# Float32 transposes in both mixtures, with the split into high and low parts moved to the read of PSUM

## The chip, the cores and the metric

The kernel runs on one core of a Trainium2 chip. The metric is the device time of one execution in microseconds; the time of a kernel is the median of its runs.

## The reference, cut to what matters

A causal convolution over 7 taps is followed by two mixtures of experts. x has 4 x 3584 = 14336 rows of 192 numbers; each mixture has 8 experts with w1 of 192 x 1024 and w2 of 1024 x 192. The inputs and the result are float32.

```
# first mixture
do_compute = (x @ w_skip) > 0;  out = x
e = argmax(xc @ w_gate);  gate = softmax(xc @ w_gate)[e]        # xc = x[do_compute]
out[do_compute] = xc + gate * (relu(xc @ w1[e]) @ w2[e])
# second mixture, on the rows that the first one gives
e = argmax(x @ w_gate2 + bias[modality]);  gate = softmax(...)[e]
out = gate * (relu(x @ w1[e]) @ w2[e])
```

## The kernel before, in words

**Stages.** The first stage (lines 353 to 746) convolves, computes the logits and writes every row, with its logits, gate and token number (202 numbers, ROW), to the bucket of its expert in a DRAM tensor. Then `mixture(0)` and `mixture(1)` (lines 751 to 1129) run one after the other. Each goes through the buckets in units of 256 rows. A segment is the run of units of one expert; its first unit (`first`) also converts the weights of the next segment, and in the first mixture computes a product with the next gate (`fold`) between the other matmuls. In this run the first mixture has 33 units in 8 segments, the second 57 units, nearly all in one segment.

**Precision.** The products are taken in fp32r, a form of float32 with fewer bits that TensorE multiplies in one pass. To keep accuracy each operand is split: a high part (the value rounded to fp32r) and a low part (value minus high part), and three of the four products are added up. `xt` holds the transposed rows of a unit in three blocks of 256 columns: block 0 the high part of columns 0 to 127 (DA = 128), block 1 the low part of the same, block 2 the last 64 columns (DB = 64), their high part in partitions 0 to 63 and their low part in partitions 64 to 127.

**One unit g**, engine by engine, each in the order written; semaphores tie them together:

- SyncE (`unit`, line 811): loads the rows of unit g+2 into `ahead` once unit g+1 was split (line 815), then the rows of unit g again into `kept` (line 822, or four columns of them in line 820) once the result buffer is free (`y_read`), and in a first unit, when the weights in `stage` were converted, the weights of the segment after the next (lines 238 to 241, 213, 214).
- ScalarE (`unit`, line 1003): four times `hid_hi`, the relu of an up product read from PSUM (line 1008), in a first unit with pieces of the weights between (line 204). After the fourth, in the first mixture only, `r_copy` (line 995 to 997) copies the finished rows of unit g-1 into `sent`; it waits until the rows sent before have landed in DRAM (`sent_done`). Then `read_xt(g+1)` (line 987) copies the transposed rows from PSUM into `xt`; then `r_exp` (line 1001) for the routing, and `rows_hi(g+2)` (line 991), the high part of the rows in `ahead`.
- VectorE (`unit`, line 1103): four times `hid_lo` (line 1106), in a first unit with low parts of weights (line 208); then in the first mixture `route` (lines 1049 to 1065) and `dest` (lines 1070 to 1075) for the rows of unit g-1, of which line 1060 (`pick`) gives what TensorE needs for the ranks; then `finish(g)` (lines 1084 to 1099), which reads the result from PSUM with the rows in `kept`.
- GpSimd (`unit`, line 872): `split_rows(g+2)`, the low parts (lines 855, 856), then the scatter of the routed rows by indirect DMA (line 862).
- TensorE (`unit`, line 950): 40 matmuls `up` (line 915) once `xt` is ready; `transpose(g+1)` (lines 904, 905, 907); 32 matmuls `down` (lines 924 and 928) in eight steps f of four; in the first mixture `r_ranks(g)` (lines 937, 939) after step 5, in a first unit after step 7. It waits for `rpick_done`, that is for line 1060.

So `transpose(g+1)` stands in the middle of unit g, and what follows it has the time of `down` before `up(g+1)` needs `xt`. `ahead`, `split` and `xt` have one buffer each.

Of the kernel before, what the change touches and what calls it, by code (L numbers as in the profile page):

```python
# [14 lines left out]
def conv_two_moes(nc, x, weight, w_skip, w_gate1, modality, w_gate2, bias2, w1, w2, w2_t, out):  # L39
# [6 lines left out]
    P = 128  # L46
# [29 lines left out]
    with ctx:  # L76
# [73 lines left out]
        ahead = sb("ahead", [P, SUBS, ROW])  # L150
        split = sb("split", [P, SUBS, 2 * D], F32R)
# [599 lines left out]
        def mixture(layer):  # L751
# [5 lines left out]
            with layer_psum:  # L757
# [3 lines left out]
                def s(name):  # L761
                    return sem(f"{name}_{layer}")

                p_h = pb("p_h", [P, HB, 512])
                p_xt = pb("p_xt", [P, 1024], F32R)
# [5 lines left out]
                rows_hi_done, split_done, xt_ready, xt_read = s("rows_hi_done"), s("split_done"), s("xt_ready"), s("xt_read")  # L771
# [30 lines left out]
                with nc.Block() as block:  # L802
                    @block.sync
                    def _(sp):
# [3 lines left out]

                        segs = sp.value_load(n_segs[layer][0:1, 0:1], min_val=2, max_val=E)

                        def unit(g, n, k, slot, first):
                            src = rows_of(g + 2)
                            sp.wait_ge(split_done, g + 2)
                            passed(sp)
                            sp.dma_start(ahead[:, :, :], src).then_inc(ahead_loaded, 16)
# [22 lines left out]
                        sp.dma_start(ahead[:, :, :], rows_of(0)).then_inc(ahead_loaded, 16)  # L838

                        load_weights(sp, sp.value_load(seg_w[layer][0:1, 1:2], min_val=0, max_val=CL - 1))  # L840
                        sp.wait_ge(split_done, 1)
                        sp.dma_start(ahead[:, :, :], rows_of(1)).then_inc(ahead_loaded, 16)
# [7 lines left out]
                    def _(pool):  # L850
                        def split_rows(g):

                            pool.wait_ge(rows_hi_done, g + 1)
                            passed(pool)
                            nc.gpsimd.tensor_tensor(split[:, :, D + DB:2 * D], ahead[:, :, 0:DA], split[:, :, 0:DA].bitcast(F32), ALU.subtract)  # L855
                            nc.gpsimd.tensor_tensor(split[:, :, D:D + DB], ahead[:, :, DA:D], split[:, :, DA:D].bitcast(F32), ALU.subtract)\  # L856
                              .then_inc(split_done, 1)

# [13 lines left out]
                        def unit(g, n, k, slot, first):  # L872
# [7 lines left out]
                            split_rows(g + 2)  # L880
# [8 lines left out]
                        split_rows(0)  # L889
                        split_rows(1)  # L890
# [8 lines left out]
                    def _(pe):  # L899
                        def transpose(g):  # L900
                            pe.wait_ge(split_done, g + 1)
                            for t in range(SUBS):
                                o = t * P
# [78 lines left out]
                    def _(act):  # L982
                        act.preload_act_table(ACT.Exp)

                        def read_xt(g):
                            act.wait_ge(xt_ready, g + 1)
                            nc.scalar.activation(xt[:, :], p_xt[:, 0:3 * UNIT].bitcast(F32), ACT.Copy).then_inc(xt_read, 1)  # L987
# [166 lines left out]
```

## Time and profile before

| | |
|---|---|
| median of 3 runs | 1263.01 us (1259.74 to 1268.81) |
| span of the profiled execution | 1261.0 us |
| mean granted TensorE clock | 0.911 of full speed |
| busy: TensorE / VectorE / ScalarE / GpSimd | 92% / 50% / 39% / 37% |
| up products, line 915 | 461.0 us |
| down products, lines 928 and 924 | 447.2 and 352.4 us |
| transposes, lines 904, 905, 907 | 43.3, 44.7 and 46.1 us |

The profile gives the span of its execution and no device time of its own beside it. Busy times of matmuls that overlap are added up by line, so the lines of TensorE sum to more than its busy time. In the profile PE is TensorE's matmuls, PEld its weight loads, DVE VectorE, ACT ScalarE, POOL GpSimd and SPq the requests that SyncE issues. "idle before <-X" is the time in which the engine had nothing to run before this instruction, and X what ended that.

### The profile page before, as it was taken

What the parts mean: (1) busy time and instruction counts of PE and PEld (TensorE: products, weight loads), DVE (VectorE), ACT (ScalarE), POOL (GpSimd) and SP (SyncE); (2) the same over time, 40 slices, a digit from 0 to 9 for tenths busy, and PEclk for the clock granted to TensorE, in tenths of its full rate; (3) what the DMA queues carried; (4) which work ended last, traced back from release to release, by engine and by line L of the source; (5) the groups of instructions that cost most, each with busy time, mean ns of one, the idle gap of its engine ahead of it and who ended that gap; (6) DMA issues with size and microseconds to landing.
All of it is one profiled execution on the core that took longest, in us unless ns stands there. A gap on an engine that the chain in (4) does not pass through costs nothing. (4 is left out here: it accounts for less than half of the span.)

```text
span 1261.0 us, 27560 instructions
## 1 busy us (share of the span) xinstructions
PE 1154.4 (92%) x8677; PEld 1134.5 (90%) x8678; DVE 625.7 (50%) x1896; ACT 489.1 (39%) x879; POOL 465.4 (37%) x576
## 2 busy tenths in 40 slices
PE   1999998289999999999982999999999999999997
PEld 1998998289999999999982999999999999999997
DVE  1356647426666666666662544444444444444444
ACT  0555545124343444444431433333333333333333
POOL 3177567612332323423331432233332332322334
PEclk7667757559999999999995999999999999999999
DMA  5244434444414334244124311111111111111110
GB/s 122 68 118 136 123 103 117 129 117 106 143 41 135 87 110 119 79 117 118 46 57 132 97 39 45 39 42 42 39 39 45 39 42 42 39 44 40 39 45 27
DMA packets 85561, 97.91 MB, mean 78 GB/s; under 512 B 26719, under 2 KB 76211, under 8 KB 85535
## 3 DMA queue, kind: packets, MB, share of 16 engines
q1 hardware_dynamic: 68362, 67.04, 20.6%
q0 software_dynamic: 15072, 28.47, 6.7%
q10 hardware_dynamic: 2100, 2.09, 0.5%
q8 instruction: 11, 0.18, 0.1%
q14 instruction: 16, 0.12, 0.0%
HBM read 65.79 MB, written 33.54 MB: 79 GB/s over the span
## 5 line engine op out<-in xcount | busy, mean ns | idle before, releaser
L915 PE MATMUL p_h<-xt,w_up 128*128 128x256 f32 x3600 | 461.0, 285 | 13.2 <-ACT xt L987 6.9
L915 PEld LDWEIGHTS p_h<-xt,w_up 128*128 128x128 f32 x3600 | 448.3, 190 | 18.4 <-ACT xt L987 9.2
L928 PE MATMUL p_y<-w_dn,hid_hi 128*128 128x384 f32 (+1 forms) x1440 | 447.2, 371 | 0.2 <-DVE hid_lo L1106 0.2
L1008 ACT ACTIVATE hid_hi<-p_h 128x512 fp32r<-128x512 f32 x360 | 215.0, 598 | 514.5 <-PE p_h L915 512.1
L924 PE MATMUL p_y<-w_dn,hid_lo 128*128 128x192 f32 (+1 forms) x1440 | 352.4, 255 | 0.0
L1106 DVE SCALAR_TENSOR_TENSOR hid_lo<-p_h,hid_hi 128x512 fp32r<-128x512 f32 x360 | 247.1, 690 | 209.2 <-ACT hid_hi L1008 208.7
L924 PEld LDWEIGHTS p_y<-w_dn,hid_lo 128*128 128x128 f32 x1440 | 275.8, 192 | 0.0
L928 PEld LDWEIGHTS p_y<-w_dn,hid_hi 128*128 128x128 f32 x1440 | 272.4, 189 | 1.2 <-DVE hid_lo L1106 0.4
L862 POOL DMA_INDIRECT out<-y_out,idx x114 | 112.3, 985 | 243.9 <-DVE y_out L1099 223.4
L855 POOL TENSOR_TENSOR split<-ahead,split 128x256 fp32r<-128x256 f32 x94 | 64.3, 684 | 300.8 <-ACT split L991 300.7
L455 POOL DMA_INDIRECT buckets<-rows,idx x128 | 125.7, 982 | 68.8 <-issue 50.3
L1092 DVE TENSOR_SCALAR y_lo<-p_y,kept 128x192 f32<-128x192 f32 x114 | 42.3, 412 | 184.2 <-PE p_y L928 184.2
L862 POOL DMA_INDIRECT buckets<-sent,idx x68 | 67.0, 985 | 73.7 <-DVE idx L1075 63.3
L904 PE MATMUL p_xt<-ident_r,split 128*128 128x128 f32 x184 | 43.3, 242 | 40.8 <-POOL split L856 40.8
L987 ACT ACTIVATE xt<-p_xt 128x768 fp32r<-128x768 f32 x92 | 73.9, 803 | 4.7 <-PE p_xt L907 4.7
L208 POOL TENSOR_TENSOR w_dn<-stage,w_dn 128x384 fp32r<-128x384 f32 x44 | 43.3, 1017 | 86.5 <-ACT w_dn L204 86.5
L568 ACT ACTIVATE rows<-p_conv 112x384 f32<-112x384 f32 x64 | 31.0, 493 | 86.4 <-PE p_conv L477 35.5
L904 PEld LDWEIGHTS p_xt<-ident_r,split 128*128 128x128 f32 x184 | 26.1, 142 | 41.3 <-POOL split L856 41.0
L479 PE MATMUL p_conv<-x_in,band 118*112 118x192 f32 x192 | 54.7, 431 | 4.7 <-ACT rows L568 4.7
L991 ACT ACTIVATE split<-ahead 128x384 fp32r<-128x384 f32 x94 | 48.9, 520 | 22.3 <-DMA ahead<-buckets 22.3
L586 ACT ACTIVATE xt<-p_xt 128x1344 fp32r<-128x1344 f32 x32 | 41.3, 1290 | 17.2 <-PE p_xt L492 17.2
L907 PE MATMUL p_xt<-ident_r,split 128*128 128x128 f32 x184 | 46.1, 250 | 0.0
(193 smaller groups left out, 1297.7 us busy)
## 6 DMA issues: line engine op xcount, KB each, us to landing
ahead<-buckets SPq DMA_DIRECT2D x94, 202.0 KB, 2.4
x_in<-in_x SPq DMA_DIRECT2D x16, 672.0 KB
stage<-in_w SPq DMA_DIRECT2D x11, 768.0 KB
kept<-buckets SPq DMA_DIRECT2D x33, 202.0 KB, 2.6
stage<-in_w SPq DMA_DIRECT2D x11, 512.0 KB
stage<-in_w SPq DMA_DIRECT2D x22, 256.0 KB
x_in<-in_w_t SPq DMA_DIRECT2D x9, 512.0 KB, 7.2
x_in<-in_w_t SPq DMA_DIRECT2D x9, 256.0 KB, 8.0
```

The lines of the kernel that those rows point to most:

```text
L455: pool.indirect_dma_start(out=buckets, out_offset=bass.IndirectOffsetOnAxis(ap=idx[:, k, t:t + 1], axis=0), in_=rows[:, k, t, :], in_offse ...
L479: mm = nc.tensor.matmul(o, band[:, head, :], x_in[0:KP, k % 2, :, cols], start=True, stop=True)
L855: nc.gpsimd.tensor_tensor(split[:, :, D + DB:2 * D], ahead[:, :, 0:DA], split[:, :, 0:DA].bitcast(F32), ALU.subtract)
L862: pool.indirect_dma_start(out=to, out_offset=bass.IndirectOffsetOnAxis(ap=place[:, t:t + 1], axis=0), in_=src[:, t, :], in_offset=None, bo ...
L904: nc.tensor.matmul(p_xt[:, o:o + P], split[:, t, 0:DA], ident_r[:, :], start=True, stop=True, is_transpose=True)
L915: mm = nc.tensor.matmul(o, w_up[:, slot, w, f * P:(f + 1) * P], xt[:, a * UNIT:(a + 1) * UNIT], start=(m == 0), stop=(m == len(terms) - 1))
L924: nc.tensor.matmul(p_y[:, t, 0:COLS], hid_lo[:, f, c], w_dn[:, slot, f, 0, 0:COLS], start=False, stop=False)
L928: mm = nc.tensor.matmul(p_y[:, t, 0:2 * COLS], hid_hi[:, f, c], w_dn[:, slot, f, :, 0:COLS], start=(f == 0), stop=(f == FT - 1))
L987: nc.scalar.activation(xt[:, :], p_xt[:, 0:3 * UNIT].bitcast(F32), ACT.Copy).then_inc(xt_read, 1)
L991: nc.scalar.activation(split[:, :, 0:D], ahead[:, :, 0:D], ACT.Copy).then_inc(rows_hi_done, 1)
L1008: nc.scalar.activation(hid_hi[:, 2 * b:2 * b + 2, :], p_h[:, b % HB, :].rearrange("p (f c) -> p f c", f=2), ACT.Relu).then_inc(hi_done, 1)
L1106: nc.vector.scalar_tensor_tensor(hid_lo[:, 2 * b:2 * b + 2, :], p_h[:, b % HB, :].rearrange("p (f c) -> p f c", f=2), 0.0, hid_hi[:, 2 * b ...
```

## The change

The transposes read `ahead` itself, in float32: columns 0 to 127 in one transpose, and a second one of 128 columns that holds the last 64 columns twice. For that `ahead` is loaded with two requests, the second of which writes the last 64 columns again behind the first copy. There are four transposes a unit in place of six. `split`, `rows_hi` and `split_rows` are gone. ScalarE reads the transposed rows into blocks 0 and 2 of `xt`, rounding to fp32r, and VectorE (`xt_lo`, two instructions) then subtracts that from what is in PSUM: into block 1, and in partitions 64 to 127 of block 2. `up(g+1)` now waits for VectorE. `xt_lo(g+1)` stands on VectorE behind the four `hid_lo` and ahead of the gate product's low part, `route`, `dest` and `finish`. SyncE waits for the transposes of unit g+1, and no longer for its split, before it loads `ahead` for unit g+2.

```diff
-        ahead = sb("ahead", [P, SUBS, ROW])
-        split = sb("split", [P, SUBS, 2 * D], F32R)
+        ahead = sb("ahead", [P, SUBS, DA + 2 * DB])
...
-                p_xt = pb("p_xt", [P, 1024], F32R)
+                p_xt = pb("p_xt", [P, 2, UNIT])
...
+                        def load_ahead(src):
+                            sp.dma_start(ahead[:, :, 0:D], src[:, :, 0:D]).then_inc(ahead_loaded, 16)
+                            sp.dma_start(ahead[:, :, D:D + DB], src[:, :, DA:D]).then_inc(ahead_loaded, 16)
...
                         def unit(g, n, k, slot, first):                      # SyncE
                             src = rows_of(g + 2)
-                            sp.wait_ge(split_done, g + 2)
+                            sp.wait_ge(xt_ready, g + 2)
                             passed(sp)
-                            sp.dma_start(ahead[:, :, :], src).then_inc(ahead_loaded, 16)
+                            load_ahead(src)
...
-                        sp.dma_start(ahead[:, :, :], rows_of(0)).then_inc(ahead_loaded, 16)
+                        load_ahead(rows_of(0))
 
                         load_weights(sp, sp.value_load(seg_w[layer][0:1, 1:2], min_val=0, max_val=CL - 1))
-                        sp.wait_ge(split_done, 1)
-                        sp.dma_start(ahead[:, :, :], rows_of(1)).then_inc(ahead_loaded, 16)
+                        sp.wait_ge(xt_ready, 1)
+                        load_ahead(rows_of(1))
...
-                            split_rows(g + 2)                                # GpSimd, and its definition
...
-                        split_rows(0)
-                        split_rows(1)
...
                         def transpose(g):
-                            pe.wait_ge(split_done, g + 1)
+                            pe.wait_ge(ahead_loaded, (g + 1) * 32)
                             for t in range(SUBS):
-                                o = t * P
-                                nc.tensor.matmul(p_xt[:, o:o + P], split[:, t, 0:DA], ident_r[:, :], start=True, stop=True, is_transpose=True)
-                                nc.tensor.matmul(p_xt[:, UNIT + o:UNIT + o + P], split[:, t, D + DB:2 * D], ident_r[:, :], start=True, stop=True,
-                                                 is_transpose=True)
-                                mm = nc.tensor.matmul(p_xt[:, 2 * UNIT + o:2 * UNIT + o + P], split[:, t, DA:DA + 2 * DB], ident_r[:, :],
-                                                      start=True, stop=True, is_transpose=True)
+                                o = slice(t * P, (t + 1) * P)
+                                nc.tensor.matmul(p_xt[:, 0, o], ahead[:, t, 0:DA], ident[:, :], start=True, stop=True, is_transpose=True)
+                                mm = nc.tensor.matmul(p_xt[:, 1, o], ahead[:, t, DA:DA + 2 * DB], ident[:, :], start=True, stop=True, is_transpose=True)
                             mm.then_inc(xt_ready, 1)
...
                         def read_xt(g):                                      # ScalarE
                             act.wait_ge(xt_ready, g + 1)
-                            nc.scalar.activation(xt[:, :], p_xt[:, 0:3 * UNIT].bitcast(F32), ACT.Copy).then_inc(xt_read, 1)
-
-                        def rows_hi(g):
-                            act.wait_ge(ahead_loaded, (g + 1) * 16)
-                            nc.scalar.activation(split[:, :, 0:D], ahead[:, :, 0:D], ACT.Copy).then_inc(rows_hi_done, 1)
+                            whole = xt[:, :].rearrange("p (h c) -> p h c", c=UNIT)
+                            nc.scalar.activation(whole[:, 0:3:2, :], p_xt[:, :, :], ACT.Copy).then_inc(xt_hi_done, 1)
...
-                            rows_hi(g + 2)
-
-                        rows_hi(0)
+
                         read_xt(0)
-                        rows_hi(1)
...
+                        def xt_lo(g):                                        # VectorE
+                            dve.wait_ge(xt_hi_done, g + 1)
+                            nc.vector.tensor_tensor(xt[:, UNIT:2 * UNIT], p_xt[:, 0, :], xt[:, 0:UNIT].bitcast(F32), ALU.subtract)
+                            tail = xt[DB:2 * DB, 2 * UNIT:3 * UNIT]
+                            nc.vector.tensor_tensor(tail, p_xt[DB:2 * DB, 1, :], tail.bitcast(F32), ALU.subtract).then_inc(xt_read, 1)
...
+                            xt_lo(g + 1)
                             if first and not last:
                                 fold_lo(dve, p_fold, 1 - slot, n + 2)
                             if not last:
...
                         nc.vector.memset(valid[:, :], 0.0).then_inc(y_read, 1)
+                        xt_lo(0)
                         segments(dve, unit)
```

## Rows read from the trace of the kernel before

**Rows 1.** Busy time by stretch: length, PE, PEld, DVE, ACT, POOL, PEclk, DMA, GB/s.

```profile
260.10:261.90 1.80, 0.03 (x2) 0.02 (x1) 0.17 (x1) 0.80 (x2) 0.73 (x2) 1.00 0.15 43
262.50:282.90 20.40, 20.40 (x86) 19.78 (x85) 6.54 (x19) 6.58 (x15) 4.96 (x6) 0.50 0.20 57
...
685.00:689.10 4.10, 3.70 (x17) 3.70 (x18) 0.00 (x0) 0.52 (x1) 0.00 (x0) 0.50 0.64 190
...
900.00:1255.00 355.00, 354.03 (x2783) 353.77 (x2781) 153.87 (x327) 128.66 (x222) 111.07 (x145) 1.00 0.14 40
```

**Rows 2.** Transposes: timeline of the weight loads; then by line, ns min/median/max.

```profile
1010.56 0.14 PEld L904 LDWEIGHTS p_xt<-ident_r,split 128*128 128x128 f32 x1
...
1011.09 0.19 PEld L928 LDWEIGHTS p_y<-w_dn,hid_hi 128*128 128x128 f32 x1
...
L904 PEld LDWEIGHTS p_xt<-ident_r,split x184: 137/141/183, 252.2 to 1248.9; 128*128 128x128 f32 x184
L904 PE MATMUL p_xt<-ident_r,split x184: 220/245/368, 252.2 to 1248.9; 128*128 128x128 f32 x184
...
L519 PEld LDWEIGHTS p_log<-ident,mod_f x1: 168/168/168, 7.5 to 7.5; 128*112 128x112 f32 x1
L519 PE MATMUL p_log<-ident,mod_f x1: 461/461/461, 7.5 to 7.5; 128*112 128x128 f32 x1
```

**Rows 3.** Waits from 230 us on: us in total, times, longest.

```profile
ACT sent L997 <- DMA buckets<-sent,idx: 43.0, 15, 7.5
...
PEld p_h L915 <- ACT xt L987: 9.2, 8, 1.8
```

**Rows 4.** Timeline, unit after a first unit: start, duration, engine, line.

```profile
324.41 0.34 SPq L815 DMA_DIRECT2D ahead<-buckets  x1
325.73 0.34 SPq L822 DMA_DIRECT2D kept<-buckets  x1
...
326.71 0.16 DVE L1049 TENSOR_SCALAR valid<-rows 128x2 f32<-128x2 f32 x1
327.88 0.17 DVE L1060 TENSOR_TENSOR pick<-hot,valid 128x16 bf16<-128x16 f32 x1
329.32 0.19 PE L937 MATMUL p_r<-pick,before 128*128 128x24 bf16 x1
330.25 0.54 ACT L997 ACTIVATE sent<-rows 128x404 f32<-128x404 f32 x1 [4.17 <-DMA buckets<-sent,idx]
330.69 0.79 ACT L987 ACTIVATE xt<-p_xt 128x768 fp32r<-128x768 f32 x1
331.54 3.86 PE L915 MATMUL p_h<-xt,w_up 128*128 128x256 f32 x30 [0.70 <-ACT xt L987]
335.61 1.46 PE L915 MATMUL p_h<-xt,w_up 128*128 128x256 f32 x10 [0.22 <-DVE hid_lo L1106]
```

**Rows 5.** The page's costliest groups, with mean ns; last, DMA issues to landing.

```profile
L1008 ACT ACTIVATE hid_hi<-p_h 128x512 fp32r<-128x512 f32 x360 | 215.0, 598 | 514.5 <-PE p_h L915 512.1
L1106 DVE SCALAR_TENSOR_TENSOR hid_lo<-p_h,hid_hi 128x512 fp32r<-128x512 f32 x360 | 247.1, 690 | 209.2 <-ACT hid_hi L1008 208.7
L1092 DVE TENSOR_SCALAR y_lo<-p_y,kept 128x192 f32<-128x192 f32 x114 | 42.3, 412 | 184.2 <-PE p_y L928 184.2
...
kept<-buckets SPq DMA_DIRECT2D x33, 202.0 KB, 2.6
```

**Rows 6.** Timeline of an ordinary unit of the first mixture.

```profile
607.59 0.81 ACT L987 ACTIVATE xt<-p_xt 128x768 fp32r<-128x768 f32 x1
...
609.07 0.17 DVE L1060 TENSOR_TENSOR pick<-hot,valid 128x16 bf16<-128x16 f32 x1
...
610.52 0.19 PE L937 MATMUL p_r<-pick,before 128*128 128x24 bf16 x1
...
611.87 0.76 DVE L1094 SCALAR_TENSOR_TENSOR y_lo<-p_y,kept 128x200 f32<-128x200 f32 x2
```

**Rows 7.** Timeline, start of the second mixture.

```profile
688.52 0.52 ACT L991 ACTIVATE split<-ahead 128x384 fp32r<-128x384 f32 x1 [4.65 <-DMA ahead<-buckets]
```

More of the change, by code:

```diff
@@ L770, in mixture @@
                 ahead_loaded, kept_loaded = s("ahead_loaded"), s("kept_loaded")
-                rows_hi_done, split_done, xt_ready, xt_read = s("rows_hi_done"), s("split_done"), s("xt_ready"), s("xt_read")
+                xt_ready, xt_hi_done, xt_read = s("xt_ready"), s("xt_hi_done"), s("xt_read")
                 h_ready, hi_done, lo_done = s("h_ready"), s("hi_done"), s("lo_done")
@@ L850, in _ @@
                     def _(pool):
[L851 to L857, printed above, removed]
                         def scatter(place, src, to):
```

## The prediction

> **What bounds the kernel now.** I read the busy times by stretch first. In the second mixture TensorE has 354.03 us of work in a stretch of 355 us, at the full clock [rows 1]: only what lies in TensorE's own order moves the time there, and work taken from ScalarE or GpSimd brings nothing. Next the table of waits, for the places where TensorE stands still. In the first mixture ScalarE waits 43.0 us in 15 places for the rows sent to DRAM, and TensorE's weight loads wait 9.2 us in 8 places for ScalarE's copy of the transposed rows [rows 3]. The two belong together, which the timeline shows [rows 4]: in the unit after a first unit the weights of a later expert fill the DMA queues, the sent rows land late, ScalarE stands 4.17 us in `r_copy`, and `read_xt` behind it starts only at 330.69. `up` starts at 331.54, 0.70 us late. This happens after each of the first seven of the eight first units (the eighth loads no weights). The eighth wait is at the start of the second mixture.
>
> **TensorE's part.** Six transposes take from 1010.56 to 1011.09, 0.53 us or 0.088 each [rows 2]. The only float32 transpose in the trace is line 519: one load and one matmul, not two as other float32 products have. Its matmul ends 461 - 168 = 293 ns after its load; at the same low clock the slowest fp32r one (a first one) ends 368 - 183 = 185 ns after [rows 2]. The difference of 108 ns is 128 columns at 1.2 GHz, so float32 takes a second clock per column. At 2.4 GHz that makes 2 x 128 / 2.4 = 107 ns, and four take about 0.45 us: 0.08 us saved a unit. Bounds: if the 0.035 us by which today's transposes exceed 128 columns at 2.4 GHz come on top, four take 0.57 us (0.04 lost); at today's 0.088 they take 0.35 (0.18 saved). I take 0.08, as line 519 is the same instruction. Over the 83 units whose time TensorE sets: **-6.6 us** (-15 to +3).
>
> The Trainium skill (TensorE: Matmul & The Clock Gate, Terms) says that the transpose mode of trn2 is four times faster for FP32. If that means the pace of fp32r, the sum would have the bound of -15 us in this place; line 519's row speaks for half that pace.
>
> **ScalarE and GpSimd.** ScalarE's read has 512 columns in place of 768: 0.60 us by line 1008 for 0.80 [rows 5]. `rows_hi` and `split_rows` go, which TensorE waits for only at the start of a mixture.
>
> **VectorE.** `xt_lo` is two instructions of 256 columns. Between 0.41 us for 192 and 0.69 for 512 columns [rows 5] each takes 0.47; with some overlap 0.9 for both. In an ordinary unit the read starts at 607.59 [rows 6] and now ends at 608.2, `xt_lo` at 609.1. `up` needs `xt` only when `finish` reads the result, at 611.87 [rows 6]: hidden by `down`, in both mixtures; without that cover it would be 0.7 a unit (0.9 more for 0.2 less). But in the first mixture `xt_lo` stands ahead of `route`, whose `pick` TensorE awaits in the middle of `down`: `route` takes 1.17 + 0.17 us to the end of `pick` (326.71 to 328.05) [rows 4], so `pick` is ready at 610.4. TensorE comes for it at 610.52 today and at 610.44 then [rows 6]. It just fits: cost 0, bounds 0 and 0.3 us in each of 18 ordinary units, +5 us at most.
>
> **The unit after a first unit** is where the change costs. There `pick` is ready at 328.05 today, before TensorE comes for it at 329.32, and only `up` has to wait for the late read [rows 4]. Now `route` stands behind `xt_lo`, that behind `read_xt`, that behind `r_copy`. The read ends at 331.3, `xt_lo` at 332.2, `pick` at 333.5. TensorE stands from 329.2 to 333.5 with two steps of `down` still to do. Today `up` could have started 1.5 us after the rank matmuls (331.54 - 0.70 - 329.32). So it starts at 335.0 in place of 331.54: 3.4 us later, in seven units: **+24 us**. The unit that follows loses today about 0.5 us because VectorE is behind with `finish` (30 matmuls take 4.07 us to 335.61, at 0.12 each they need 3.6 [rows 4]); with `up` later this goes: **-3.5 us**.
>
> This rests on the order of the queue. The Trainium skill (TensorE: Matmul & The Clock Gate, Part 1, Architectural detail) says that TensorE pulls only weight loads ahead and keeps its matmuls in program order, and that ScalarE and VectorE are strict FIFO. By that rule nothing of `down` slips past the rank matmuls and the 24 us stand; if it could, only the 0.7 us by which `xt` comes later would be left, 5 us in seven units. The trace agrees as far as it goes: no matmul of `down` is seen ahead of ranks that stand before it.
>
> **The clock.** The new stalls last 4.3 us or more. At 260.10:261.90 TensorE is idle for 1.8 us at clock 1.00, and 262.50:282.90 then runs at 0.50 although it is busy throughout [rows 1]. The stalls of today's seven units, 0.7 to 1.8 us, leave the clock high. So I expect a fall after nearly every new stall. In 685.00:689.10, dense `up` at 0.50, 17 matmuls take 3.70 us [rows 1] where 2.1 would do at 0.12 each: 1.6 us lost before the clock is back at 689. I take 2.0 each, six times: **+12 us** (0 to 7 x 3 = 21).
>
> **SyncE.** The load of `ahead` leaves half a unit earlier than needed, as before; a second request costs the queue about 0.6 us. `kept` now waits behind both. It follows `ahead` by 1.3 us when nothing holds it (324.41 to 325.73) [rows 4] and lands in 2.6 [rows 5]. The transposes end about half a microsecond before the read at 607.59, so `kept` lands at 607.1 + 0.2 + 0.6 + 1.3 + 2.6 = 611.8, and `finish` reads it at 611.87 [rows 6]. In the second mixture `finish` may begin 0.5 us later. Its cover is the next `up`, 5 us; without it, 0.5 a unit. Weights are requested after the same waits as before: 0.
>
> **Start of the second mixture.** ScalarE stands in `rows_hi(1)` until `ahead` lands at 688.52 [rows 7] before it may read the first `hid_hi`; this wait goes, and the first transposes need no split (1.5 us less in the chain, against 0.6 for the second request and 0.7 for `xt_lo`). **-2 us** (0 to -4). In the first mixture the start waits for the gate product's operand anyway: 0.
>
> **Sum** against the span of 1261.0: -6.6 + 24 - 3.5 + 12 - 2 = +24, 1285. The median of the runs lies 2 us above that span; with the same distance the median after is **1287 us**.
>
> **Rivals.** (A) *The wait for the ranks comes, the clock stays high.* For: today's stalls of up to 1.8 us in these units did not lower it. Against: the fall after 1.8 us at 261.9. Sum without 12: **1275**. (B) *Faster.* The sent rows land early: the loads of `ahead` and `kept` at 324.41 and 325.73 are no longer requested beside them. If they land 4.17 us earlier, ScalarE's read is done before TensorE asks for ranks; the new wait is gone, and today's 9.2 us too: -6.6 - 9 - 3.5 - 2 = -21, **1242**. It decides once the rows land over 4 us sooner. Against: in SyncE's order those two stand behind the requests for the weights, so they can hardly have held anything up. (C) *The float32 transposes go in two passes of two clocks*, as other float32 products do: eight of 0.107 a unit, 0.86 in place of 0.53 us, 83 times 0.33 = +27 in place of -6.6: **1321**. Line 519 is a single instruction, which speaks against it. (D) *The ordinary units of the first mixture wait too*, 0.3 us each in 18, and the clock falls in all seven, 3 us each: +5 and +9 more: **1301**.
>
> **Chances.** Forecast 0.55; A 0.2; B 0.08; C 0.03; D 0.14. Two runs of one kernel differ by up to about 1%, which is what a measurement can tell from no change: 12.6 us. Slower by more holds the forecast, C, D and a quarter of A: 0.77. Same: most of A, 0.16. Faster: B, 0.07. The range runs from A with a somewhat larger saving on transposes, 1269, to D, 1303; it leaves out B and C.
>
> **What would show it.** In the profile after: PE L937's line has "idle before" of about 30 us in seven places, each over 4 us, released by DVE `pick`; the wait of PE L915 for `xt` is nearly gone; the clock row shows dips in the first mixture; the second mixture has units of 9.84 us and no idle. The prediction is wrong if those seven stalls are absent, if the transposes' four loads take over 0.57 us, or if the clock stays at 1.00.

## The result, and the profile after

The kernel after takes **1298.51 us** (median of 4 runs, 1294.43 to 1304.26), the kernel before 1263.01: the ratio is 1.0289 (95% interval 1.0244 to 1.0334). A later comparison gave 1.0277 (1.0217 to 1.0337). The forecast of 1287 us had the sign and most of the way there, and the range (1269 to 1303) holds the time; 11.5 us are missing from the point. The profiled execution took 1300.72 us, its span is 1299.0.

The busy time by stretch comes first, as before. The columns are those of [rows 1]; the first fence is of the kernel after, the second, a stretch that the rows ahead of the prediction don't have, of the kernel before.

```profile
282.95:661.83 378.88, 337.85 (x2443) 328.82 (x2441) 230.11 (x794) 125.85 (x255) 80.05 (x82) 0.94 0.33 94
900.00:1255.00 355.00, 355.00 (x2743) 355.00 (x2742) 183.28 (x397) 104.04 (x181) 70.82 (x74) 1.00 0.18 47
293.75:300.58 6.83, 6.29 (x30) 6.28 (x31) 3.96 (x17) 0.60 (x1) 1.96 (x2) 0.50 0.09 30
338.13:341.54 3.41, 3.41 (x17) 3.39 (x16) 2.28 (x10) 0.00 (x0) 1.53 (x2) 0.50 0.08 27
```

```profile
282.95:661.83 378.88, 366.39 (x2822) 356.79 (x2819) 240.14 (x853) 160.47 (x319) 126.83 (x158) 1.00 0.34 97
```

The second mixture is full as before. The first is not: in the same stretch TensorE works 338 us where it had 366, and its clock is 0.94 on average for 1.00. Both short stretches are at half clock: they begin at the end of a stall (the first 0.5 us before it, the second 0.6 us after it), and TensorE is busy in all the rest. There are seven such, 44.4 us in all.

What TensorE waits for is in the table of waits from 230 us on (line waited, us in total, times, longest), with other waits that changed:

```profile
DVE idx L1044 <- DMA kept<-buckets: 168.4, 57, 5.6
...
DVE xt L1065 <- ACT xt L954: 65.6, 36, 6.6
...
ACT sent L960 <- DMA buckets<-sent,idx: 41.5, 8, 6.9
PE p_r L903 <- DVE pick L1020: 38.5, 8, 6.3
...
PE p_h L881 <- issue: 6.0, 7, 1.2
```

The wait of the weight loads of `up` for `read_xt` (9.2 us in 8 places, [rows 3]) is gone in the first mixture; at the start of the second `up` now waits 2.4 us for VectorE's part of `xt`. The ranks' wait for the pick has come: 38.5 us in 8 places, of which 3.48 at the end of the mixture stood there before (3.22). Seven others make 35.0 us, 3.99 to 6.31 each (forecast: about 30, each over 4). The last row, seven waits of `up` for "issue", is one that the prediction does not have.

The second unit of this kind shows the chain. This is the timeline of the kernel after; it answers to [rows 4].

```profile
333.26 0.26 PE L890 MATMUL p_y<-w_dn,hid_lo 128*128 128x200 f32 x1
334.15 0.54 ACT L960 ACTIVATE sent<-rows 128x404 f32<-128x404 f32 x1 [3.94 <-DMA buckets<-sent,idx]
334.60 0.58 ACT L954 ACTIVATE xt<-p_xt 128x512 fp32r<-128x512 f32 x1
335.21 0.42 DVE L1065 TENSOR_TENSOR xt<-p_xt,xt 128x256 fp32r<-128x256 f32 x1 [4.28 <-ACT xt L954]
335.65 0.43 DVE L1067 TENSOR_TENSOR xt<-p_xt,xt 64x256 fp32r<-64x256 f32 x1
336.11 0.17 DVE L1009 TENSOR_SCALAR valid<-rows 128x2 f32<-128x2 f32 x1
...
337.28 0.17 DVE L1020 TENSOR_TENSOR pick<-hot,valid 128x16 bf16<-128x16 f32 x1
...
337.51 0.19 PE L903 MATMUL p_r<-pick,before 128*128 128x24 bf16 x1 [3.99 <-DVE pick L1020]
```

Read it downward: the sent rows land, ScalarE copies, then reads `xt`; VectorE writes the low half; then `route`; then TensorE, idle since 333.52, may go on. Every link is as forecast. The ordinary unit and the transposes, also of the kernel after, answer to [rows 6] and [rows 2]:

```profile
356.55 0.59 ACT L954 ACTIVATE xt<-p_xt 128x512 fp32r<-128x512 f32 x1
...
359.25 0.18 DVE L1020 TENSOR_TENSOR pick<-hot,valid 128x16 bf16<-128x16 f32 x1
...
359.48 0.10 PEld L903 LDWEIGHTS p_r<-pick,before 128*128 128x128 bf16 x1 [0.18 <-DVE pick L1020]
```

```profile
1048.71 0.14 PEld L873 LDWEIGHTS p_xt<-ident,ahead 128*128 128x128 f32 x1
1048.81 0.14 PEld L874 LDWEIGHTS p_xt<-ident,ahead 128*128 128x128 f32 x1
1048.92 0.14 PEld L873 LDWEIGHTS p_xt<-ident,ahead 128*128 128x128 f32 x1
1049.03 0.14 PEld L874 LDWEIGHTS p_xt<-ident,ahead 128*128 128x128 f32 x1
1049.14 0.19 PEld L894 LDWEIGHTS p_y<-w_dn,hid_hi 128*128 128x128 f32 x1
```

The pick comes just as TensorE's matmuls do, and the four transposes take 1049.14 - 1048.71 = 0.43 us, 0.108 each.

**Where the 38.0 us went** (1299.0 - 1261.0), by the distance from the first `up` matmul of a unit to that of the next:

```
                                             before    after  difference
start, to unit 1                             282.87   280.81    -2.1
7 units after a first unit                    80.05   114.45   +34.4
7 first units (of units 3 to 29)             106.41   105.84    -0.6
the other 17 units of 1 to 31                178.16   189.47   +11.3
unit 32, and the change of mixture            37.92    36.81    -1.1
unit 33                                       12.55    11.39    -1.2
units 34 to 88 (9.92, then 9.85 each)        546.00   541.57    -4.4
last unit to the end                          17.04    18.68    +1.6
```

### The profile page after: what moved, and what is told of

It is laid out like the page before. It is cut to its first block and busy times, and to the rows that moved or that the text cites. A ratio compares the mean times of both kernels' runs of the same rounds, so it can differ in the third digit from the quotient of the medians.

```text
span 1299.0 us, 27192 instructions
## 1 busy us (share of the span) xinstructions
PE 1160.5 (89%) x8493; PEld 1140.0 (88%) x8494; DVE 697.7 (54%) x2080; ACT 431.1 (33%) x785; POOL 363.1 (28%) x388
## 2 busy tenths in 40 slices
DMA packets 123161, 103.12 MB, mean 79 GB/s; under 512 B 52286, under 2 KB 113810, under 8 KB 123134
## 5 line engine op out<-in xcount | busy, mean ns | idle before, releaser
L881 PE MATMUL p_h<-xt,w_up 128*128 128x256 f32 x3600 | 467.6, 289 | 10.2 <-issue 6.0
L881 PEld LDWEIGHTS p_h<-xt,w_up 128*128 128x128 f32 x3600 | 458.1, 197 | 13.4 <-issue 7.8
L894 PE MATMUL p_y<-w_dn,hid_hi 128*128 128x384 f32 (+1 forms) x1440 | 455.6, 376 | 0.0
L1044 DVE TENSOR_SCALAR idx<-kept 128x2 int32<-128x2 f32 x57 | 10.3, 180 | 168.4 <-DMA kept<-buckets 168.4
L873 PE MATMUL p_xt<-ident,ahead 128*128 128x128 f32 x184 | 46.7, 280 | 37.0 <-DMA ahead<-buckets 37.0
L1065 DVE TENSOR_TENSOR xt<-p_xt,xt 128x256 fp32r<-128x256 f32 x92 | 38.5, 418 | 65.6 <-ACT xt L954 65.6
L454 PE MATMUL p_conv<-x_in,band 118*112 118x192 f32 x192 | 60.4, 465 | 4.6 <-ACT rows L543 4.6
L873 PEld LDWEIGHTS p_xt<-ident,ahead 128*128 128x128 f32 x184 | 26.2, 142 | 37.4 <-DMA ahead<-buckets 37.2
L954 ACT ACTIVATE xt<-p_xt 128x512 fp32r<-128x512 f32 x92 | 54.3, 591 | 9.0 <-PE p_xt L874 9.0
L454 PEld LDWEIGHTS p_conv<-x_in,band 118*112 118x112 f32 x192 | 44.2, 254 | 7.3 <-ACT rows L543 6.6
L561 ACT ACTIVATE xt<-p_xt 128x1344 fp32r<-128x1344 f32 x32 | 41.3, 1290 | 18.7 <-PE p_xt L467 18.7
L874 PE MATMUL p_xt<-ident,ahead 128*128 128x128 f32 x184 | 46.1, 277 | 0.0
```

Source lines behind the costliest of these rows:

```text
L454: mm = nc.tensor.matmul(o, band[:, head, :], x_in[0:KP, k % 2, :, cols], start=True, stop=True)
L873: nc.tensor.matmul(p_xt[:, 0, o], ahead[:, t, 0:DA], ident[:, :], start=True, stop=True, is_transpose=True)
L874: mm = nc.tensor.matmul(p_xt[:, 1, o], ahead[:, t, DA:DA + 2 * DB], ident[:, :], start=True, stop=True, is_transpose=True)
L881: mm = nc.tensor.matmul(o, w_up[:, slot, w, f * P:(f + 1) * P], xt[:, a * UNIT:(a + 1) * UNIT], start=(m == 0), stop=(m == len(terms) - 1))
L894: mm = nc.tensor.matmul(p_y[:, t, 0:2 * COLS], hid_hi[:, f, c], w_dn[:, slot, f, :, 0:COLS], start=(f == 0), stop=(f == FT - 1))
L954: nc.scalar.activation(whole[:, 0:3:2, :], p_xt[:, :, :], ACT.Copy).then_inc(xt_hi_done, 1)
```

## The experiments

Each ratio is to the kernel before, run beside it on the same chip. In the first group of four (before_wait, pick_first, read_first, before_read_first) the kernel before itself took 1300.63 us, not 1263. The first stage took longer there: in the four traces unit 0 starts at 290 to 295 us, elsewhere at 250 to 257. Why is not shown. Expectations of this group that name absolute times are therefore read as ratios or differences. In the second group it took 1262.52, in the third 1264.30.

The same ledger for all traces, in us:

```
                     7 after first   other 17   units 1-32   one unit of   last unit
                                                             mixture 2     to the end
before                    80.05       178.16      402.5         9.92         17.0
after                    114.45       189.47      446.6         9.85         18.7
before_wait              108.27       182.48      434.9         9.94         17.0
before_read_first         72.75       185.70      401.9         9.92         17.0
read_first                72.42       185.55      400.0         9.85         18.7
pick_first                83.70       175.07      400.6         9.85         18.6
kept_first               112.83       187.06      442.1         9.85         16.2
ranks_late                98.41       195.29      438.9         9.82         18.7
pick_and_read             71.73       178.71      392.1         9.85         17.8
all_three                 71.89       178.50      392.5         9.85         16.2
before_both               71.97       184.64      400.5         9.92         17.1
after_again              110.76       189.79      443.2         9.85         18.7
transposes_twice         110.93       188.14      441.7        10.29         18.7
all_again                 71.46       178.34      391.7         9.85         16.2
```

The rows after and after_again are two executions of the same kernel. They differ by 3.7 us in the first column (and by 6.1 us in the time up to unit 1, which is not in this table), so a difference of that size between two traces says nothing by itself.

**The wait alone, in the kernel before.** Nothing but the new order of waits is added: VectorE may not route before `xt` of the next unit has been read.

```diff
                             if not last:
+                                if not first:
+                                    dve.wait_ge(xt_read, g + 2)
                                 route(g)
```

> The kernel before the change with one wait added: in the units of the first mixture that are no first units, VectorE waits for the read of the transposed rows of the next unit ahead of route. No transposes, loads or splits are changed. Theory: this alone makes most of the loss. pick follows the late read by 1.4 us, seven stalls of about 3.6 us, a fall of the clock after each, 27 us in the units themselves and 5 us in those after them, 1285 to 1298. The rivals (SyncE's requests, float32 transposes) expect no loss beyond what a bare wait costs: 1261 to 1268.

It took 1331.46 us beside 1300.63: ratio 1.0236 (1.0202 to 1.0271). One line of waiting, with the old transposes, reproduces 2.36 of the 2.89%. Here are the wait of the second such unit and the clock in the stretch that begins 0.6 us before the end of this wait:

```profile
372.63 0.20 PE L937 MATMUL p_r<-pick,before 128*128 128x24 bf16 x1 [3.88 <-DVE pick L1060]
```

```profile
372.04:378.87 6.83, 6.24 (x29) 6.23 (x30) 4.46 (x17) 0.97 (x2) 3.04 (x4) 0.50 0.30 88
```

The seven stalls last 2.88 to 4.73 us. A fall comes with six of them; with the shortest, 2.88 us, it does not. This kernel has none of the new transposes, so they are not needed for the clock to fall.

**The pick ahead of `xt_lo`** (VectorE, first mixture, units that are not first):

```diff
-                        def route(g):
+                        def route(g, between=None):
...
                             nc.vector.tensor_tensor(q3(pick1), q3(hot), spread(valid[:, :]), ALU.mult).then_inc(rpick_done, 1)
+                            if between:
+                                between()
...
-                            xt_lo(g + 1)
+                            if first or last:
+                                xt_lo(g + 1)
...
-                                route(g)
+                                route(g, None if first else lambda: xt_lo(g + 1))
```

> In the units of the first mixture that are no first units, xt_lo(g+1) moves behind pick on VectorE; all else as in the changed kernel. Theory (the order on VectorE: ranks wait for pick, pick for xt_lo, xt_lo for the late read, and the clock falls in that stall): pick is ready 2.8 us after the transposes begin, the seven waits of TensorE before the rank matmuls are gone, the clock stays at 1.00 through the first mixture, and the small waits before the first units (0.6 to 1.2 us, line 881, issue) go too. up then waits for the late xt, about 0.75 us more than before the change in seven units. Span 1257 to 1262, median 1259 to 1264. Rival 1 (SyncE's later requests and the two loads of ahead): nothing of them is changed here, so 1290 or more. Rival 2 (float32 transposes pull the clock down): four of them a unit are still there, the falls stay, 1280 or more.

**ScalarE reads `xt` ahead of `r_copy`** (same units):

```diff
-                                if not last and b == NB - 1:
+                                if first and not last and b == NB - 1:
                                     r_copy(g)
...
                             read_xt(g + 1)
+                            if not first and not last:
+                                r_copy(g)
```

> In the units of the first mixture that are no first units, ScalarE reads the transposed rows ahead of r_copy; VectorE keeps the order of the changed kernel. Theory: xt_lo no longer hangs on the rows sent to DRAM, pick is ready about 3.5 us after the transposes begin in every such unit, so the seven stalls and the falls of the clock go, and with them the 0.9 to 1.7 us that up waited for xt already before the change. Span 1244 to 1250, median about 1248: faster than both kernels. If the stalls come from SyncE's requests or from the transposes themselves, they stay: 1280 or more.

Ratios: pick_first 0.9972 (0.9956 to 0.9989), read_first 0.9939 (0.9918 to 0.9960). Either cut of the chain turns the loss of 2.9% into a small gain, and no wait ahead of the ranks is left in either until the mixture's end. pick_first gained 4.8 us, where up to 4 were expected, though the clock still fell once, for 3.4 us. read_first gained 8 us, where 13 to 19 were expected. (Nine of its ten executions took 1289.99 to 1297.83 us; one took 5782.41, and nothing here shows why.) What remains differs. In pick_first `up` still has to wait for `xt`, as in the kernel before and longer: six waits of 1.6 to 2.1 us at this place.

```profile
368.70 6.55 PE L881 MATMUL p_h<-xt,w_up 128*128 128x256 f32 x40 [1.78 <-DVE xt L1069]
```

In read_first that goes too (72.4 us for the seven units), but the pick stays behind `xt_lo`, and the waits for "issue" ahead of first units remain (4.5 us, waits of the trace of read_first, 325 to 690 us):

```profile
PE p_h L881 <- DVE hid_lo L1074: 5.2, 5, 2.1
PE p_h L881 <- issue: 4.5, 7, 0.9
```

**The same order of ScalarE in the kernel before:** the edit of read_first.

> The kernel before the change with r_copy behind the read of the transposed rows on ScalarE in the units of the first mixture that are no first units. It tells how much of a gain of the same edit in the changed kernel is the edit's own. Theory: the waits of up for xt in seven units (8 us together) and what follows them (4 us) go: 1249 to 1253, some 4 us above the changed kernel with the same edit. If the late read is not what up waits for, 1261 to 1264.

Ratio 0.9956 (0.9927 to 0.9985). The seven units after a first one go from 80.05 to 72.75 us; the units behind them give back 7.5 us, because VectorE's `finish` is late instead and `up` waits in its middle for `hid_lo`. By the medians the order gains 6.5 us, half of the 10 to 14 expected; by this ledger hardly any of that lies in the first mixture (402.5 and 401.9 us). The traced execution took 1300.55 us, 6.5 above its median, so its trace may not show the gain; where it lies is open. So ScalarE's order cost the kernel before little; the late copy came to matter when the ranks were tied to it.

**SyncE asks for `kept` first:**

```diff
                         def unit(g, n, k, slot, first):
-                            src = rows_of(g + 2)
-                            sp.wait_ge(xt_ready, g + 2)
-                            passed(sp)
-                            load_ahead(src)
                             src = rows_of(g)
                             sp.wait_ge(y_read, g + 1)
...
+                            src = rows_of(g + 2)
+                            sp.wait_ge(xt_ready, g + 2)
+                            passed(sp)
+                            load_ahead(src)
...
                         segments(sp, unit)
+                        sp.wait_ge(ahead_loaded, (total(sp) + 2) * 32)
+                        passed(sp)
```

> The changed kernel, with SyncE asking for the unit's kept rows ahead of the rows of two units on, in place of behind them. Theory (ranks wait for the pick, pick for xt_lo, xt_lo for read_xt, read_xt for the sent rows): the seven waits ahead of the ranks stay, 4 to 6 us each; only the tail of the second mixture, where the finish waits 2.4 us for kept rows, gets about 1.5 us shorter, so the time is 1 to 2 us under the changed kernel (ratio to it 0.997 to 1.001). Rival (SyncE's queue: kept rows held up by the wait for the transposed rows pace the units): most of the 57 waits of VectorE for kept rows, 5.6 us each, end in shorter units, and the time falls by 15 us or more.

The changed kernel was measured beside it:

> The changed kernel itself, once more, as the one that the others of this group are compared with. Its first comparison gave 1.0289 of the kernel before. The runs so far show the kernel before at 1300.63 us here and at 1263.01 us in the first session, the difference lying in the first stage; if the first stage is all that differs, the loss stays about 36 us and the ratio is 1.028 (1.022 to 1.033).

after_again 1300.30 us, 1.0277 (1.0217 to 1.0337); kept_first 1297.17, 1.0272 (1.0214 to 1.0330). The two cannot be told apart, and the seven stalls are still there (3.6 to 5.3 us), so SyncE's order is not the cause. It is a good case of a large wait that costs nothing. In the kernel after, VectorE waits 168.4 us in 57 places for `kept`. In kept_first (740 to 1290 us) that wait is replaced by one for the matmuls:

```profile
DVE y_lo L1054 <- PE p_y L896: 130.6, 53, 2.5
...
DVE idx L1046 <- DMA kept<-buckets: 5.8, 1, 5.8
```

and the unit stays at 9.85 us. Only the last unit, with no next `up` to cover it, is shorter: 16.25 for 18.68 us.

**Float32 transposes issued twice** (second mixture only):

```diff
-                            for t in range(SUBS):
+                            for t in list(range(SUBS)) * (2 if last else 1):
```

> The changed kernel, with each of the four float32 transposes of a unit issued twice in the second mixture, and once in the first, as before; the output is the same. It measures what these transposes cost on TensorE where nothing else ends the unit. By the spacing of four transposes and the next weight load in the trace (0.43 us a unit), 57 units of the second mixture get 0.43 us longer each: 24.5 us over the changed kernel (units of 10.28 us for 9.85), ratio to it about 1.019. If float32 transposes cost no more than the two-byte ones of before (0.088 us a step), it is 20 us; if each took 0.14 us, 32 us. If the clock fell because of them, the granted clock in the second mixture, 1.00 now, would fall and the loss would be over 40 us.

1326.00 us beside after_again's 1300.30, ratio of the medians 1.0198. Units 34 to 88 take 565.77 in place of 541.57 us: 0.440 a unit, 0.110 a transpose. (The old transposes, which the expectation calls two-byte ones, are fp32r.) The load of each of the eight follows the last by 0.10 to 0.11, and the clock stays up:

```profile
1049.47 0.14 PEld L873 LDWEIGHTS p_xt<-ident,ahead 128*128 128x128 f32 x1
...
1050.23 0.14 PEld L874 LDWEIGHTS p_xt<-ident,ahead 128*128 128x128 f32 x1
1050.34 0.19 PEld L894 LDWEIGHTS p_y<-w_dn,hid_hi 128*128 128x128 f32 x1
```

```profile
740.00:1300.00 560.00, 560.00 (x4357) 560.00 (x4356) 281.74 (x599) 163.28 (x273) 107.49 (x110) 1.00 0.19 48
```

**The ranks always at the end of `down`:**

```diff
-                                if not last and f == (FT - 1 if folds else 5):
+                                if not last and f == FT - 1:
```

> The changed kernel, with TensorE's rank matmuls always behind the last down matmuls of the unit, not behind the sixth of ten. The pick comes at T+8.5 us as before, but four steps of down (2.4 us with the slow clock) are done while TensorE waits. Theory: the seven units after a first one lose 2.1 to 2.4 us each (16 us in all), the wait ahead of the ranks goes from 5.0 to about 3.2 us, and the 0.6 to 1.2 us ahead of the seven first units mostly go, since nothing holds TensorE's sequencer in the middle of down: 15 to 22 us under the changed kernel, ratio to the kernel before 1.010 to 1.016. Rival (the pick is not what TensorE waits for): no wait gets shorter.

1292.73 us, ratio 1.0222 (1.0184 to 1.0261), where the changed kernel had 1.0289 and 1.0277: a gain of some 8 us, half of what was expected. The seven units behave as forecast, 114.45 to 98.41 us (2.3 each), with stalls of 2.3 to 4.05 us ahead of the ranks (3.4 on average), and the clock still falls after each. Against after_again (110.76) the seven gain 1.8 each. The rest of the expectation was wrong. Behind the sixth step stand two more steps of `down`, not four. The waits ahead of first units do not go: they are 0.7 to 1.8 us now, the other 17 units take 5.8 us more, and one first unit 1.5 us more. To move the rank matmuls does not shorten these waits. They go with the pick, which comes 3.99 to 4.53 us after the first transpose, where the changed kernel has 4.0: `up` follows its end by 2.1 or 2.6 us in each of the seven places, against 2.2 or 2.7.

**All three orders together,** and without SyncE's:

> The changed kernel with three orders changed: ScalarE reads xt ahead of the copy that waits for the sent rows (units other than a first one, first mixture), VectorE picks ahead of xt_lo in the same units, and SyncE asks for kept rows first. The first two alone gave 0.9939 and 0.9972 of the kernel before. Theory: each of the two takes away the same link, so together they give hardly more than the better one, and the tail 1 us besides: 0.990 to 0.995 of the kernel before, no wait ahead of the ranks, no fall of the clock after them. Rival (the two links cost separately and add): 0.985 or less.

> all_three without SyncE's order. Against all_three it shows what SyncE's order is worth: by the two tails (16.24 and 18.7 us) 2.4 us, and nothing in the units. Ratio to the kernel before 0.986 to 0.988; the first mixture takes 392 to 394 us from unit 1 to unit 33, the seven units after a first one 10.2 us each, and those ahead of a first one 10.1 to 10.4 us (11.0 to 11.5 in the changed kernel).

> all_three once more, on the chip and beside the runs of the others of this group, for a second comparison with the kernel before. The first gave 0.9852 (0.9797 to 0.9908). Ledger by stages: first mixture 10 us shorter than in the kernel before, second 4.4, tail 0.8, start 0 to 2: 15 to 17 us in all, ratio 0.986 to 0.988.

all_three 1245.69 us, 0.9852 (0.9797 to 0.9908), and again 1250.97, 0.9888 (0.9855 to 0.9921); pick_and_read 1250.80, 0.9884 (0.9838 to 0.9930). It beats both kernels: 1.1 to 1.5% under the kernel before, about 4% under the change as it was made. I had expected hardly more than read_first alone (0.9939), which was wrong; the rival, that the two add up, had 0.985 or less. The two cuts do more together, since each removes what the other leaves: the seven units take 71.9 us, as in read_first, and the other 17 take 178.5, not 185.6. In all_three ScalarE still waits 4.12 us for the sent rows, but nothing of TensorE's stands behind it:

```profile
328.04 0.59 ACT L956 ACTIVATE xt<-p_xt 128x512 fp32r<-128x512 f32 x1
332.74 0.54 ACT L962 ACTIVATE sent<-rows 128x404 f32<-128x404 f32 x1 [4.12 <-DMA buckets<-sent,idx]
```

```profile
333.42 0.17 DVE L1028 TENSOR_REDUCE den<-expd 128x2 f32<-128x16 f32 x1 [2.51 <-ACT expd L966]
```

```profile
337.12 1.46 PE L883 MATMUL p_h<-xt,w_up 128*128 128x256 f32 x10 [0.76 <-DVE hid_lo L1078]
```

```profile
288.00:652.00 364.00, 359.18 (x2745) 352.06 (x2744) 252.97 (x897) 140.76 (x287) 89.99 (x92) 1.00 0.38 104
```

That is the chain as it now stands (ScalarE, VectorE, TensorE, and TensorE's stretch): the late sent rows hold `r_exp` behind `r_copy`, VectorE's `den` waits 2.51 us for it, `finish` and so `hid_lo` are late, and TensorE loses 0.76 us in place of 3.99. The clock stays at 1.00. SyncE's order makes no difference that can be measured: 0.9884 without, 0.9888 with it (in the traces the last unit takes 17.8 and 16.2 us).

**What the change is worth in the right order:** the kernel before with the edits of before_read_first and kept_first. It has the six old transposes and the splits ahead of them, so it prices both together.

> The kernel before (two-byte-step transposes, rows split ahead of them) with two of the three orders of all_three: ScalarE reads xt ahead of the copy that waits for the sent rows, SyncE asks for kept rows first. It shows what the float32 transposes are worth once the orders are right. The first order alone gave 0.9956 of the kernel before; its ordinary and second-mixture units stay as before (10.19 and 9.92 us), so against all_three it should be longer by 55 x 0.073 = 4 us in the second mixture, about 3 us in the first and 2 us at its start: 8 to 11 us over all_three, ratio to the kernel before 0.990 to 0.996. If float32 transposes are worth nothing, it equals all_three (0.985).

1258.67 us, 0.9959 (0.9934 to 0.9984), beside 1250.97 for all_again: the medians differ by 7.7 us, and the intervals of the two ratios do not meet. By the ledger the old way costs 4.2 us in the second mixture (0.076 x 55), where TensorE's own transposes set the time, and 8 to 9 in the first. Of the latter some 3 us are `up` waiting for `hid_lo` (7.3 us in all in before_both, 4.4 and 4.5 in all_again and all_three), which is not the transposes' own time. 2.3 us come back at the start, which scatters by more than that from run to run.

## Why the prediction was right, and where it fell short

**Order of the queues: shown.** before_wait gives the loss without the change, pick_first and read_first take it away with the change in place. The term was 24 us. In the seven units the ranks come 35.35 us later than before, and 7.80 us between ranks and next `up`, the waits of the kernel before, go: **27.5**. Nearly all of the difference lies in three units in which the sent rows landed 0.7 to 2.1 us later than before (`r_copy` at 6.06, 5.94 and 7.06 us after the first transpose, before 4.97, 5.24 and 4.99). That is scatter between executions and not the change: worked out in the same way, the traces of after_again, kept_first and transposes_twice give 24.3, 24.9 and 23.2. So the term was right, and its 3.5 us too much in this trace are not a lasting part of the loss. The change also moves `ahead` in more and shorter packets (123161 of all queues, 52286 of them under 512 bytes, for 85561 and 26719). The rows did not land later for it: the mean of the seven `r_copy` is 5.26 us in the trace before and 5.51 in before_wait, both without these packets, and 5.74, 5.29, 5.36 and 5.13 in after, after_again, kept_first and transposes_twice.

**Following unit: -3.5 forecast, -4.2 found** (`up` to the first transpose, 5.37 us before, 4.78 undisturbed). **Clock: 12 forecast, 15.8 found.** It fell after all seven stalls, not six. With the slow clock the rest of `down` behind the ranks takes 2.0 to 2.44 us in place of 1.38 (7.0 us in all), and the `up` of the next unit 8.8 us more in all: 2.3 a fall, where I took 2.0 from the one fall of the old trace. The clock was low for 3.4 or 6.8 us each time; six of the seven falls began 0.5 to 2.2 us before the end of the stall, while TensorE had nothing to do. Rival A (the clock stays high) is out, and B (the sent rows land early) too: they landed no earlier. Of D a part came true: all seven falls, and a little of the ordinary units.

**Transposes: the pace was right, the term was not.** Line 519 foretold 0.107 us; 0.108 is read off and 0.110 measured by doubling. The Trainium skill (TensorE: Matmul & The Clock Gate, Terms) calls the transpose mode of trn2 four times faster for FP32. Read as fp32r's pace, that is not borne out on this chip: a float32 transpose takes 0.110 us where the fp32r one took 0.088. Two passes (rival C) are out as well. The second mixture got 4.4 us shorter (0.081 x 55) as forecast. In the first mixture only the first units gained (0.6 us in all); ordinary ones went from 10.19 to 10.21 us, where pick_first and all_three have 10.10. The 0.1 us is what the pick's being just in time costs: I called that 0, with bounds of 0 and 0.3. The term comes to about -5 in place of -6.6.

**The missed step: TensorE's own sequencer, +6.4 us.** The prediction counted the pick as in time when it comes with TensorE's matmuls, and priced nothing behind. But seven first units now start 0.63 to 1.17 us late, for "issue":

```profile
369.69 0.10 PEld L903 LDWEIGHTS p_r<-pick,before 128*128 128x128 bf16 x1 [0.19 <-DVE pick L1020]
...
370.85 0.36 PE L894 MATMUL p_y<-w_dn,hid_hi 128*128 128x400 f32 x1
372.38 2.41 PE L881 MATMUL p_h<-xt,w_up 128*128 128x256 f32 x18 [1.17 <-issue]
```

From the end of the pick, 369.64, to `up` it is 2.7 us, though `down` ends at 371.2. Between two experts the sequencer ends one loop, loads registers (`segments` reads the segment's bounds, lines 765 and 766) and enters the next. In its order the ranks' wait for the pick stands ahead of this work. The trace of the kernel after has these instructions; PEldq is TensorE's sequencer, and the columns are ns min/median/max, then first and last start (stretch 300 to 660 us):

```profile
L765 PEldq TENSOR_LOAD <-seg_start x7: 302/303/308, 307.6 to 653.1; - x7
L766 PEldq TENSOR_LOAD <-seg_start x7: 297/298/307, 308.3 to 653.9; - x7
```

In all seven places its first instruction stands 0.06 us behind the end of the pick. The last stands 2.1 us behind it, or 2.6 where the outer loop over pairs of segments also closes (every second time), and `up` follows 0.1 us later. So `up` cannot start sooner than 2.2 or 2.7 us after the pick. With an early pick the sequencer does this while queued matmuls run. The runs bear it out, since the wait grows as the pick gets later while the distance stays:

```
                     pick after the first   `up` after the pick   wait for "issue"
                     transpose, us
before_wait               3.40                2.2 or 2.7             0.04 to 0.08, or 0.58 to 0.61
read_first                3.67                2.2 or 2.7             0.42 to 0.44, or 0.93 to 0.95
after                     4.00                2.2 or 2.7             0.63 to 0.65, or 1.15 to 1.17
ranks_late                3.99 to 4.53        2.1 or 2.6             0.72 to 1.05, or 1.47 to 1.79
```

With the pick early (2.78 us, in pick_first, pick_and_read and all_three) the two kinds of units ahead of a first one take 10.10 and about 10.37 us, as the kernel before's 10.19 and 10.46, not 11.01 and 11.5. The 0.1 us for "issue" that is left in the longer kind stood in the kernel before too.

**SyncE and `kept`: right in the units** (9.85 us, forecast 9.84), short at the end: `finish` of the last unit has no next `up` to cover it, **+1.6**. **Start of the second mixture: -2 forecast, -2.3 found** (units 32 and 33). The start of the first is 2.1 us shorter in this trace and 4 us longer in after_again, which is the same kernel, so it is scatter and not the change's.

The sum: -5.0 + 27.5 - 4.2 + 15.8 - 2.3 + 6.4 + 1.6 - 2.1 = 37.7 of 38.0. The main mechanism and its size were right. That the range held was partly luck: its upper end was made for 0.3 us in each of 18 ordinary units, which came to 0.1, and not for the sequencer, which took that room; one of the four executions (1304.26) lies above it.

## What to carry to other kernels

When a change puts an instruction into an in-order queue, follow everything behind it to the unit in which what it waits for is latest, not to the average one: 1 us of VectorE work that was hidden in ordinary units tied the ranks to a DMA and cost 43 us there with the clock (27.5 and 15.8). The seven stalls of 4.0 to 6.3 us, 35.0 in all, cost 15.8 us more in clock, nearly half as much again. "Just in time" is late for an engine whose sequencer has its own work to do beyond the wait; and the cure was not to drop the change but to move two calls, after which it is worth 7.7 us, about the 8.6 that the forecast gave to the transposes and the start of the second mixture.

## What the runs showed of the hardware that I had not expected

A semaphore that is set just as TensorE's matmuls reach it can cost 0.6 to 1.2 us some 1.5 us later, at the next change of loop, with nothing in the table of waits but "issue": behind the wait the sequencer has 2.1 or 2.6 us of its own work there, two register loads of 0.30 us among it. The stalls of 2.97 us and more ahead of the ranks of these units each came with 3.4 or 6.8 us of half clock; the one of 2.88 us did not. Of the thirteen stalls of 1.61 to 2.47 us ahead of `up` or the ranks in the first mixtures of all the runs, six did (one each in pick_first, read_first, before_read_first and before_both, two in ranks_late). A float32 transpose of 128 by 128 costs 0.110 us on TensorE, an fp32r one 0.088; VectorE subtracts 128x256 from PSUM in 0.42 us, where I had interpolated 0.47.
